# Attention and two MLPs on one core: in the slots without MLP TensorE makes the memory's norms, and loads go out at other ticks

## The reference, cut to what matters

```
scores = q @ k.T / 8, causal; a = exp(scores - max); a /= a.sum() + 1e-9
local = a @ v
q_p = where(q > 0, q, exp(q) - 1) + 1                      # phi
mem_out = (q_p @ M_prev) / ((q_p * z_prev).sum(-1) + 1e-6) # retrieval and its norm
x = g * mem_out + (1 - g) * local,  g = sigmoid(beta) per head
h = x @ w_in;  x = piecewise(h) @ w_out                    # MLP 1: 0, ((h+1)/2)^2 or h
h = x @ w_in2; out = max(0.01 h, h) @ w_out2               # MLP 2
```

## Time and profile before

| | us |
|---|---|
| runs, median of 3 (1007.44 to 1010.01) | 1008.76 |
| the profiled execution, its own time | 1010.12 |
| its span, first to last instruction | 1008.2 |
| TensorE busy in the span | 988.6 (98%) |
| VectorE, ScalarE, POOL busy | 449.2, 513.5, 429.2 |

### The profile page before, as it was taken

The page is one execution under the profiler, slowest core; times in us unless marked ns, Lnnn a source line. Parts: engine busy times, 40 slices in busy tenths (PEclk is TensorE's granted clock), DMA queues, the critical chain, the costliest instruction groups (busy, mean ns, idle before and its releaser), DMA issues.

```text
span 1008.2 us, 16616 instructions
## 1 busy us (share of the span) xinstructions
PE 988.6 (98%) x6174; PEld 867.2 (86%) x6174; DVE 449.2 (45%) x1110; ACT 513.5 (51%) x1111; POOL 429.2 (43%) x382
## 2 busy tenths in 40 slices
PE   7799999999999999999999999999999999999998
PEld 5688899998999999999999998888888888888897
DVE  5768766766666656666521266212122121211111
ACT  6677768676767677676633475223222222222221
POOL 2568655656464554646332287222222222222222
PEclk9999999999999999999999999999999999999999
DMA  7773233323323333323111264001000200100010
GB/s 206 181 201 97 62 78 71 83 67 79 79 65 84 77 70 81 81 59 83 41 23 42 82 209 129 21 1 36 28 21 1 63 21 1 55 8 1 1 43 21
DMA packets 100112, 66.77 MB, mean 66 GB/s; under 512 B 76096, under 2 KB 89664, under 8 KB 100032
## 3 DMA queue, kind: packets, MB, share of 16 engines
q1 hardware_dynamic: 98720, 61.26, 24.2%
q10 hardware_dynamic: 1312, 4.46, 1.3%
HBM read 54.53 MB, written 11.08 MB: 65 GB/s over the span
## 4 chain that ended last, share of the span: by engine, by line
PE 87%; DVE 4%; DMA 3%; ACT 2%; SPq 2%; issue 2%; POOL 1%; DVEq 0%; POOLq 0%; ACTq 0%
PE Hp L677 12%; PE Hp L676 12%; PE Hp L675 12%; PE Yp L699 7%; PE Yp L700 7%; PE Yp L705 6%; PE At L705 6%; PE At L699 6%; PE At L700 6%; PE At L601 4%; PE At L626 4%; PE At L538 3%; PE At L586 1%; DMA raw<-short 1%; DMA rn<-PTl_raw 1%
## 5 line engine op out<-in xcount | busy, mean ns | idle before, releaser
L1307 POOL TENSOR_TENSOR Gl<-Gl_raw,Gh 128x512 fp32r<-128x512 f32 x144 | 191.4, 1329 | 435.4 <-ACT Gh L918 435.4
L675 PE MATMUL Hp<-Xh,WAh 128*128 128x256 f32 (+1 forms) x704 | 214.7, 305 | 1.8 <-DVE Xl L1135 1.1
L676 PE MATMUL Hp<-Xl,WAh 128*128 128x256 f32 (+1 forms) x704 | 212.7, 302 | 0.0
L677 PE MATMUL Hp<-Xh,WAl 128*128 128x256 f32 (+1 forms) x704 | 212.6, 302 | 0.0
L1151 DVE TENSOR_TENSOR Gl_raw<-Hp,Gl_raw 128x512 f32<-128x512 f32 x72 | 49.8, 691 | 297.5 <-ACT Gl_raw L910 297.5
L910 ACT ACTIVATE Gl_raw<-Hp 128x512 f32<-128x512 f32 x72 | 43.1, 598 | 230.5 <-PE Hp L677 230.5
L675 PEld LDWEIGHTS Hp<-Xh,WAh 128*128 128x128 f32 x704 | 134.0, 190 | 10.3 <-DVE Xl L1135 1.3
L676 PEld LDWEIGHTS Hp<-Xl,WAh 128*128 128x128 f32 x704 | 134.2, 191 | 7.8
L918 ACT ACTIVATE Gh<-Gl_raw 128x512 fp32r<-128x512 f32 x144 | 90.9, 631 | 94.7 <-DVE Gl_raw L1151 52.2
L677 PEld LDWEIGHTS Hp<-Xh,WAl 128*128 128x128 f32 x704 | 134.0, 190 | 4.9
L699 PE MATMUL Yp<-WBh,Gh 128*128 128x512 f32 x320 | 132.6, 415 | 0.6 <-DVE WBl L1130 0.6
(11 more groups left out here) (144 smaller groups left out, 1928.7 us busy)
## 6 DMA issues: line engine op xcount, KB each, us to landing
raw<-long SPq DMA_DIRECT2D x16, 480.0 KB, 4.4
WAl_raw<-w_in SPq DMA_DIRECT2D x12, 512.0 KB, 5.0
WBl_raw<-w_out SPq DMA_DIRECT2D x12, 512.0 KB, 4.4
Vs_raw<-v_long SPq DMA_DIRECT2D x16, 320.0 KB, 3.5
yT_scratch<-xraw SPq DMA_DIRECT2D x36, 128.0 KB, 2.5
prob<-yT_scratch SPq DMA_DIRECT2D x9, 512.0 KB, 4.6
out<-prob SPq DMA_DIRECT2D x34, 128.0 KB, 2.2
raw<-short SPq DMA_DIRECT2D x11, 384.0 KB, 4.2
```

Source lines behind the costliest of these rows:

```text
L675: pe.matmul(h, WAh[:, f, j, :], xh, start=(j == 0), stop=False)
L676: pe.matmul(h, WAh[:, f, j, :], xl, start=False, stop=False)
L677: last = pe.matmul(h, WAl[:, f, j, :], xh, start=False, stop=(j == DT - 1))
L1307: gp.tensor_tensor(Gl[:, U % 2, :], act[:, U % 2, :], Gh[:, U % 2, :].bitcast(F32), ALU.subtract).then_inc(g_lo, 1)
```

## The change

In slots 0 to 5 TensorE makes the norms a second time behind `memory(n)`: phi is the stationary operand (128 queries, or 64, by 64 channels), one column of z the moving one, so that each norm comes out on its query's partition, in columns 448 to 450 of banks 2 and 3 of `At`. `factors` reads them from there (`norm_in`) instead of waiting for a cut, and they go out in the rows of `rt`, with the sums; `cut_norms` and `send_norms` are no longer called there, and `spread_factors` takes both from these rows. TensorE's norms(n) wait for `norm_in` of slot n-1, and the transposes into these banks wait for `norm_in` of their slot. From slot 6 on the norms go as before. SP loads the rows of slot 8 at tick 4 of slot 6, and from slot 7 on those of n+2 at tick 7 of slot n, ahead of that tick's sends. POOL makes `v_low(8)` at tick 1 instead of 0, behind the WAl tile of tick 0.

```diff
--- before.py
+++ after.py
@@ -68,6 +68,10 @@
 
 SUMS, SUMS_AT = 3 * P, [64, 128]
 RN = 16
+
+
+NORM_TILES = [(0, 128), (128, 128), (256, 64)]
+NORM_COLS, NORM_AT = 448, [6, 11]
 
 
 def part(n):
@@ -230,7 +234,7 @@
         q_min, phi_exp, phi_done = sem("q_min"), sem("phi_exp"), sem("phi_done")
         s_done, max_done, p_exp = sem("s_done"), sem("max_done"), sem("p_exp")
         mem_done, mem_out, mem_left, mem_scaled = sem("mem_done"), sem("mem_out"), sem("mem_left"), sem("mem_scaled")
-        n_cut, rn_sum, rn_inv, rn_gated, norms_sent, sums_sent, factors_in = (sem(x) for x in ("n_cut", "rn_sum", "rn_inv", "rn_gated", "norms_sent", "sums_sent", "factors_in"))
+        n_cut, norm_zero, norm_done, norm_in, rn_sum, rn_inv, rn_gated, norms_sent, sums_sent, factors_in = (sem(x) for x in ("n_cut", "norm_zero", "norm_done", "norm_in", "rn_sum", "rn_inv", "rn_gated", "norms_sent", "sums_sent", "factors_in"))
         rt_out = sem("rt_out")
         t_done, pt_hi, pt_lo = sem("t_done"), sem("pt_hi"), sem("pt_lo")
         pv_done, x_part, x_sum, x_scaled, x_done, tail_stored, tail_in = (sem(x) for x in ("pv_done", "x_part", "x_sum", "x_scaled", "x_done", "tail_stored", "tail_in"))
@@ -360,6 +364,9 @@
                 if n <= PLAIN:
                     after(sp, phi_done, n - 1)
                     after(sp, mem_done, n - 1)
+                    after(sp, norm_done, min(n - 1, OPENING))
+                    if n > OTHER_BANKS:
+                        sp.wait_ge(s_done, n - 1)
                 else:
                     sp.wait_ge(phi_done, n)
                     sp.wait_ge(q_lo, split_before(n))
@@ -388,7 +395,7 @@
             def send_norms(n):
                 w = QL[part(n)] // D
                 sp.wait_ge(rn_gated, n + 1)
-                after(sp, norms_sent, 16 * n)
+                after(sp, norms_sent, 16 * (n - OPENING))
                 at = SUMS_AT[part(n)]
                 sp.dma_start(rn_rows[n, 1, :, at:at + w * D].rearrange("h (p i) -> p h i", p=D),
                              rnr[0:D, 6:16].rearrange("p (h i) -> p h i", h=2)[:, :, 0:w]).then_inc(norms_sent, 16)
@@ -401,13 +408,18 @@
             def spread_factors(n):
 
                 at = SUMS_AT[part(n)]
-                sp.wait_ge(norms_sent, 16 * n + 16)
+                after(sp, norms_sent, 16 * (n - OPENING + 1))
                 sp.wait_ge(sums_sent, 16 * n + 16)
                 after(sp, factors_in, 32 * n)
                 after(sp, x_done, n - 1 if n <= PLAIN else n)
                 for h in range(2):
-                    sp.dma_start(bc_place(n)[D * h:D * h + D, :, 0:QL[part(n)]],
-                                 rn_rows[n, :, h, at:at + QL[part(n)]].partition_broadcast(D)).then_inc(factors_in, 16)
+                    if n < OPENING:
+                        first = SUMS // P * h * P + at
+                        step = NORM_AT[h] * P - first
+                        rows = rn_dram[n, 0, first:first + 2 * step].rearrange("(s q) -> s q", s=2)[:, 0:QL[0]]
+                    else:
+                        rows = rn_rows[n, :, h, at:at + QL[part(n)]]
+                    sp.dma_start(bc_place(n)[D * h:D * h + D, :, 0:QL[part(n)]], rows.partition_broadcast(D)).then_inc(factors_in, 16)
 
             def store_tail(n):
                 sp.wait_ge(x_done, n + 1)
@@ -423,8 +435,9 @@
 
             def slot(n, k):
                 front, back, last = stage(n)
-                if k == 0 and front is not None and OPENING + 2 <= front + 1 < SLOTS:
-                    load_qkm(front + 1)
+
+                if k == (4 if n == OPENING else 7) and front is not None and front + 2 < SLOTS:
+                    load_qkm(front + 2)
                 if k == (5 if n == OPENING else 2) and last is not None:
                     store_tail(last)
                 if k == 3 and front is not None:
@@ -441,8 +454,6 @@
 
             def opening(n):
                 front, back, last = stage(n)
-                if n != 1:
-                    cut_norms(front)
                 if n < OPENING - 2:
                     load_qkm(front + 2)
                 if back is not None:
@@ -450,9 +461,6 @@
                 if n >= OPENING - 2:
                     load_qkm(front + 2)
                 load_v(front + 1)
-                if n == 0:
-                    cut_norms(1)
-                send_norms(front)
                 send_sums(front)
                 if last is not None:
                     store_tail(last)
@@ -550,6 +558,7 @@
                 if n < OTHER_BANKS:
                     after(pe, max_done, tiles_before(n))
                 else:
+                    pe.wait_ge(norm_in, OPENING)
                     pe.wait_ge(x_sum, values_before(n - 1))
                     pe.wait_ge(pt_lo, low_before(n - 1))
                     pe.wait_ge(mem_out, n)
@@ -586,9 +595,23 @@
                         last = pe.matmul(memory_bank(n)[:, h, :], mt[r, :], ft[r, 0:ql], start=(step == 0), stop=(step == len(steps) - 1))
                 return last
 
+            def norms(n):
+
+                pe.wait_ge(norm_zero, 1)
+                after(pe, x_sum, values_before(n - 1))
+                after(pe, norm_in, n)
+                for i, (q0, count) in enumerate(NORM_TILES):
+                    for h in range(2):
+                        r, z = slice(D * h, D * h + D), D - D * h
+                        last = pe.matmul(At[0:count, 2 + h, NORM_COLS + i:NORM_COLS + i + 1], phi[r, q0:q0 + count],
+                                         memory_rows(raw_place(n), n)[r, z:z + 1], start=True, stop=True)
+                last.then_inc(norm_done, 1)
+
             def transposes(b, h, n):
                 pe.wait_ge(p_exp, tiles_before(b) + NT[part(b)] * (h + 1))
                 if h == 0:
+                    if b < OPENING:
+                        pe.wait_ge(norm_in, b + 1)
                     after(pe, x_sum, values_before(b))
                     if n >= OTHER_BANKS:
                         pe.wait_ge(max_done, tiles_before(min(n + 1, SLOTS)))
@@ -627,22 +650,24 @@
                                              start=(j == 0 and pt is PTh), stop=(j == len(blocks) - 1))
                     last.then_inc(pv_done, 1)
 
-            def keep_warm(times):
+            def keep_warm(times, bank):
 
                 for _ in range(times):
-                    pe.matmul(At[:, 3, 0:S - P], mask[:, 0:P], mask[:, 0:S - P], start=True, stop=True)
+                    pe.matmul(At[:, bank, 0:S - P], mask[:, 0:P], mask[:, 0:S - P], start=True, stop=True)
 
             def slot(n, k):
                 front, back, _ = stage(n)
                 if k == 0 and front is not None:
                     scores(front)
                     if front == 1:
-                        keep_warm(5)
+                        pe.wait_ge(mem_out, 1)
+                        keep_warm(5, 1)
                 if k == 2 and front is not None and front < OTHER_BANKS:
                     after(pe, pt_lo, low_before(front - 1))
                     memory(front).then_inc(mem_done, 1)
                     if front == 0:
-                        keep_warm(3)
+                        keep_warm(3, 3)
+                    norms(front)
                 if k in (3, 4) and back is not None:
                     transposes(back, k - 3, n)
                 if k == 5 and back is not None:
@@ -707,7 +732,8 @@
                     last.then_inc(y_done, 1)
 
             pe.wait_ge(consts0, 2)
-            keep_warm(6)
+            pe.wait_ge(norm_zero, 1)
+            keep_warm(6, 3)
             pe.wait_ge(consts_ready, 2)
             for g in range(G_END):
                 slot(g // 8, g % 8)
@@ -1016,10 +1042,17 @@
 
             def factors(n):
                 ve.wait_ge(p_exp, tiles_before(n + 1))
-                ve.wait_ge(n_cut, 32 * n + 32)
                 after(ve, sums_sent, 16 * n)
-                after(ve, norms_sent, 16 * n)
-                ve.tensor_tensor(rnr[:, 0:RN], rn[:, :], rn_tiny[:, :], ALU.add).then_inc(rn_sum, 1)
+                if n < OPENING:
+                    ve.wait_ge(norm_done, n + 1)
+                    ve.tensor_scalar(rnr[:, 6:RN].rearrange("p (h i) -> p h i", h=2)[:, :, 0:len(NORM_TILES)],
+                                     At[:, 2:4, NORM_COLS:NORM_COLS + len(NORM_TILES)], 1e-6, None, ALU.add).then_inc(norm_in, 1)
+                    ve.tensor_tensor(rnr[:, 0:6], rn[:, 0:6], rn_tiny[:, 0:6], ALU.add).then_inc(rn_sum, 1)
+                    ve.wait_ge(norm_in, n + 1)
+                else:
+                    ve.wait_ge(n_cut, 32 * (n - OPENING + 1))
+                    after(ve, norms_sent, 16 * (n - OPENING))
+                    ve.tensor_tensor(rnr[:, 0:RN], rn[:, :], rn_tiny[:, :], ALU.add).then_inc(rn_sum, 1)
                 ve.wait_ge(rn_sum, n + 1)
                 ve.reciprocal(rnr[:, 0:RN], rnr[:, 0:RN]).then_inc(rn_inv, 1)
                 ve.wait_ge(rn_inv, n + 1)
@@ -1033,6 +1066,7 @@
                 ve.wait_ge(qkm_in[odd(n)], loads(n))
```

(7 more changed lines are left out.)

## The result

| | before | changed |
|---|---|---|
| median of 5 runs, us | 1009.65 (1007.44 to 1010.29) | 1004.04 (1003.64 to 1004.71) |
| span of the profiled execution | 1008.2 | 1002.2 |
| first MLP matmul | 46.76 | 43.84 |
| TensorE busy in the span | 988.6 | 991.3 |

The ratio is 0.9949, with a 95% interval of 0.9938 to 0.9961: 5.6 us between the medians, 6.0 between the two spans. It is faster, as forecast (1003.2 us, range 1001.0 to 1006.4).

A forecast was written before the change was run, and what follows sets the result against it. TensorE was taken as the bound behind 116 us, with earlier waits behind the norms' DMAs and loads. Gains of 2.6 + 1.7 + 1.3 = 5.6 us against the 1008.76 median gave 1003.2 us, range 1001 to 1006.4.

The forecast's parts named there:

- Opening, 2.6 us: Slots 0 to 5: without the norms' DMAs the first MLP matmul comes at 44.1 us instead of 46.8.
- factors(0) at 11.05 us: VectorE, slot 0: factors starts after the last exponential's sum, at 11.05 instead of 13.09 us, 2.0 us earlier.
- scores(2) at 16.4: TensorE, slot 2: scores start at 16.4 instead of 17.71 us, 1.3 us left after norms and transposes.
- Norms at 0.84 us a slot: TensorE, opening: six added one-column matmuls, priced as three tiles like the scores' 64-column tile, 0.28 us each.
- TensorE is now the bound of the opening: Opening from scores(2): TensorE's own work sets 6.85 us a slot, four slots 27.4 us.
- it fits in 6.85: Opening: the factors-to-factors loop, 6.06 us in slot 3, fits in TensorE's 6.85 us even with the read and later transposes.
- Loads, 1.7 and 1.3 us: Earlier loads end VectorE's waits: 1.7 us of TensorE's idle time from slot 8's load, 1.3 from later loads and v_low.
- I take 1.3 us: Loads from slot 7 on, with v_low(8) moved: 1.3 us gained of TensorE's 1.47 us idle in 104 to 116 us.
- The 0.64 us for v_low's tick: POOL, making the last WAl tile before v_low(8), was to save 0.64 us, within the 1.47.
- Only the loads pay: Rival, chance 0.17: norms and waits eat the opening's gain at 7.5 us per slot; 3.0 to 3.4 us gained, 1005.5.
- Slower: Rival, chance 0.05: norms run record after record at up to 3.2 us a slot, giving 1015 us.
- More than forecast: Rival, chance 0.12: one-column matmuls hide in neighbours' weight loads, period 6.3 us, another 2 us gained: 1001.2.

The follow-up runs named there:

- the seven starts: MLP starts of the seven traced executions with the changed kernel's own opening, one with late WBl tiles: 43.43 to 44.55 us, mean 44.04.
- loads-only run: Kernel before with only the moved loads and v_low(8) at tick 1, norms by cuts: span 1005.5 us, ratio to before 0.9979.
- the run with the cuts: Changed kernel with the norms' cuts issued again and factors waiting for them, sends left out: MLP start 46.78 us, span 1006.4.

## Why the prediction was right, and where it was off

**The bound and the waits.** Right. The norms' DMAs stood before VectorE's row maxima and the loads before its minima; both waits went, and the gain stopped at slot 10, from where TensorE is bound by its own work.

**Opening, 2.6 us.** Measured 2.92 in the profiled pair, and 2.7 for the mean of the seven starts against 46.76. The loads-only run, whose opening is that of before, started its MLP at 46.39, so by the two traces of the old opening its gain is 2.4 to 2.7 us. The steps:

- factors(0) at 11.05 us: 10.98. factors(3) at 30.9: 31.30. Xl of slot 3 at 43.7: 43.79.
- scores(2) at 16.4: 16.09, since the transposes and values of slot 1 ran with one small wait behind the norms.
- Norms at 0.84 us a slot: 0.64, and a slot grew by 0.54 only, from the 5.88 of the earlier trace rows to 6.42. The 64-column tile of the scores (0.28 us for both heads) was too dear a neighbour, since a norms' tile takes 0.21. Made twice they add 0.75.
- "TensorE is now the bound of the opening", 6.85 us for each slot: wrong for half the slots, and none had the period of 6.7 to 7.0 us that was to show it. Two slots took 6.42 us and two 7.45, in which VectorE's operations beside POOL's were long. The sum was 27.75 instead of 27.4 us, so two errors cancelled; that is luck. The step that went wrong is "it fits in 6.85": the loop from `factors` to `factors` was taken from slot 3, 6.06 us. The one ahead of it, 26.02 to 33.50 in the earlier trace rows, had taken 7.48 us with no wait for a DMA in it, already more than 6.85, with the 0.99 us minimum beside POOL. In the changed kernel the loops from `factors(2)` on took 8.20, 6.58 and 7.57 us. That POOL makes these operations of the opening long is read from the timelines; only the WBl tiles of slot 9 were tested by a run.

**Loads, 1.7 and 1.3 us.** The first was too small: slot 7 gained 2.2 us, 0.5 more than the idle time that the profile shows. The rest is busy time of the same matmuls: from memory(7) to memory(8) the profile has 113 matmul records in both kernels, 17.29 us busy before and 16.76 after. The second is the other step that failed: "I take 1.3 us" for slots 8 and 9 against 0.9 measured, and in slot 9 TensorE's idle time shrank by only 0.3 of 1.47. The forecast named nothing as late next there. What was: three WBl tiles of VectorE, moved by the removed wait to where POOL works, took 4.91 us instead of 2.98, more than the 1.59 us that were freed. The 0.64 us for v_low's tick were not there either.

**The rivals.** "Only the loads pay" (7.5 us a slot) described slots 4 and 5 and not 2 and 3, which is why it failed. "Slower" needed norms of 2.0 us a slot; they are a third of that. "More than forecast" has some truth in slots 2 and 3. The Trainium skill's 2.0 us for a DMA (DMA: Bandwidth & Descriptors, Anatomy of one DMA, a fit for DMAs that GpSimd issues, while SP issues the cuts) would have had slot 0 gain nothing; it gained 2.1 us at `factors`. With the cuts put back, the wait in slot 0 was 1.0 us, not 2.83: the cut's time is not a constant of this kernel. What sets it was not measured.

**The number.** 5.6 us forecast, 5.6 between the medians, 6.0 between the spans. Term by term it was 2.6, 1.7 and 1.3 us against 2.9, 2.2 and 0.9, so that the sum fits so closely is luck in part. The forecast time, 1003.2 us, is 0.8 below the measured 1004.04: it started from 1008.76, the median of three runs, and that of five is 1009.65.

## What to carry to other kernels

When a wait is removed from an in-order engine, what stood behind it moves in time: look at which engine works beside it at the new time, and take its durations from rows with that neighbour. The loop to compare with is the longest that the trace shows without the wait, not the shortest. A delay can cost more than its size: an operation of 16 columns that came 0.03 us behind POOL's split took 2.37 us. A handful of small matmuls can be cheaper than a DMA that turns a layout, in a stage where TensorE has idle time; price them from the whole slot, not from the record alone. And ask of every load what it queues behind in its issuing engine: one load issued earlier gave 2.8 us to slot 10 (with v_low's tick), about as much as the norms gave the opening.

## What was not expected of the hardware

- VectorE's subtraction of two 128x512 operands: 0.68 us with POOL idle, 1.5 to 1.8 beside POOL; one POOL instruction put elsewhere shortened three such tiles from 4.91 to 4.09 us.
- VectorE's multiplication of 128x16: 0.17 us, and 2.37 us when it started 0.03 us behind POOL's split of 128x1024 in the run with the cuts.
- TensorE's granted clock fell to 0.50 in 18 to 20 us of the loads-only run, whose opening is that of before, and to 0.75 over 22 to 26 us in the run with the cuts. The profiled execution of before, with a wait of 1.96 us in slot 1 where the loads-only run had 1.80, kept 1.00.
- The start of the MLP varies by 1.1 us (43.43 to 44.55) among executions of the same opening, all of it outside slots 2 and 3, which take 6.42 us each time.
